# Running product on one Trainium2 core: where the square root's table is loaded, and where the second router's columns are copied

## What is computed

```python
mag = np.sqrt(a_re * a_re + a_im * a_im)
scale = np.minimum(mag, 0.999) / (mag + 1e-06)
a_re_n, a_im_n = (a_re * scale, a_im * scale)
for t in range(S):
    S_re, S_im = (ar * S_re - ai * S_im + kv, ar * S_im + ai * S_re)   # ar, ai: the decay of step t
    y[:, :, t] = np.einsum('bhd,bhde->bhe', q[:, :, t], S_re)
```

## Time and profile before

| | |
|---|---|
| three runs, median (lowest to highest) | 805.1 us (803.31 to 806.18) |
| profiled execution, its own time | 804.9 us |
| its span, first to last instruction | 803.0 us |
| mean granted TensorE clock | 0.951 |
| busy: PE, DVE, ACT, POOL | 700.5, 657.8, 476.1, 212.9 us |

### The profile page before, as it was taken

The page is one execution under the profiler, slowest core; times in us unless marked ns, Lnnn a source line. Parts: engine busy times, 40 slices in busy tenths (PEclk is TensorE's granted clock), DMA queues, the critical chain, the costliest instruction groups (busy, mean ns, idle before and its releaser), DMA issues.

```text
span 803.0 us, 17480 instructions
## 1 busy us (share of the span) xinstructions
PE 700.5 (87%) x6568; PEld 622.4 (78%) x6568; DVE 657.8 (82%) x1241; ACT 476.1 (59%) x660; POOL 212.9 (27%) x184
## 2 busy tenths in 40 slices
PE   0577867169999999947999999999999999999997
PEld 0323332158888888847999998998999999999997
DVE  7998999989999999967888767756898696676672
ACT  7678988566676676552656544646544545544541
POOL 3000000031111111105153566532344322233422
PEclk9888989579999999977999999999999999999999
DMA  7463643017853332455666866776565755756630
GB/s 192 152 216 124 207 161 109 0 34 147 158 145 101 108 118 89 166 116 177 203 220 202 278 222 205 238 222 219 192 216 180 265 192 191 245 208 188 245 139 30
DMA packets 90900, 136.85 MB, mean 170 GB/s; under 512 B 22474, under 2 KB 70070, under 8 KB 90656
## 3 DMA queue, kind: packets, MB, share of 16 engines
q1 hardware_dynamic: 83680, 119.54, 47.9%
q0 software_dynamic: 7168, 16.64, 5.8%
HBM read 124.15 MB, written 14.01 MB: 172 GB/s over the span
## 4 chain that ended last, share of the span: by engine, by line
PE 47%; DVE 4%; DMA 2%; issue 1%; ACT 1%; POOL 0%; POOLq 0%; SPq 0%; DVEq 0%
PE banks L1385 23%; PE banks L1342 22%; PE banks L1328 2%; DVE mix_spot L1578 1%; DVE w_lo L972 1%; DMA raw<-w1b 1%; DMA mix_rows<-xbuf,lists 1%; DVE mix_hT_lo L1677 0%; DMA xbuf<-mix_y,to_scatter 0%; PE banks L1320 0%; ACT mix_hT_hi L1425 0%; DVE mix_y L1701 0%; ACT w_hi L961 0%; POOL to_scatter L1218 0%; POOLq L1091 0%
## 5 line engine op out<-in xcount | busy, mean ns | idle before, releaser
L1342 PE MATMUL banks<-mix_xT_hi,w_hi 128*128 128x240 f32 x576 | 158.8, 276 | 0.6 <-DVE mix_xT_lo L1686 0.6
L1342 PE MATMUL banks<-mix_xT_lo,w_hi 128*128 128x240 f32 x576 | 158.9, 276 | 0.0
L1342 PE MATMUL banks<-mix_xT_hi,w_lo 128*128 128x240 f32 x576 | 158.8, 276 | 0.0
L1385 PE MATMUL banks<-w_hi,mix_hT_hi 128*128 128x384 f32 (+3 forms) x384 | 135.7, 353 | 3.8 <-DVE mix_hT_lo L1677 3.8
L1385 PE MATMUL banks<-w_lo,mix_hT_hi 128*128 128x384 f32 (+3 forms) x384 | 129.8, 338 | 0.0
L1385 PE MATMUL banks<-w_hi,mix_hT_lo 128*128 128x384 f32 (+3 forms) x384 | 129.7, 338 | 0.0
L1425 ACT ACTIVATE mix_hT_hi<-banks 128x480 fp32r<-128x480 f32 x96 | 54.8, 572 | 111.0 <-PE banks L1342 106.0
L1342 PEld LDWEIGHTS banks<-mix_xT_hi,w_hi 128*128 128x128 f32 x576 | 109.5, 190 | 0.9 <-issue 0.8
L1342 PEld LDWEIGHTS banks<-mix_xT_hi,w_lo 128*128 128x128 f32 x576 | 109.6, 190 | 0.0
L1342 PEld LDWEIGHTS banks<-mix_xT_lo,w_hi 128*128 128x128 f32 x576 | 109.5, 190 | 0.0
L1677 DVE SCALAR_TENSOR_TENSOR mix_hT_lo<-banks,mix_hT_hi 128x480 fp32r<-128x480 f32 x96 | 62.7, 653 | 50.5 <-ACT mix_hT_hi L1425 50.4
(11 more groups left out here) (230 smaller groups left out, 1469.0 us busy)
## 6 DMA issues: line engine op xcount, KB each, us to landing
raw<-w1b SPq DMA_DIRECT2D x16, 1536.0 KB, 7.9
raw<-w2b SPq DMA_DIRECT2D x16, 1536.0 KB
A<-w2a_t SPq DMA_DIRECT2D x8, 1536.0 KB, 8.4
raw<-w1a SPq DMA_DIRECT2D x8, 1536.0 KB
raw<-w2a SPq DMA_DIRECT2D x8, 1536.0 KB
ring<-a SPq DMA_DIRECT2D x9, 864.0 KB, 5.1
qk<-q SPq DMA_DIRECT2D x48, 96.0 KB, 2.3
qk<-k SPq DMA_DIRECT2D x48, 96.0 KB, 2.3
```

What stands on the lines that cost most here:

```text
L1342: last = pe.matmul(pU[g % TURNS][:, n * N:(n + 1) * N], w1p[m][:, b, c, f * P:(f + 1) * P], xT[s][:, c, 0:N], start=(c == 0 and (s, m) == ...
L1385: last = pe.matmul(pD[0:m, half, 0:ph.width], hT[s][:, f, half * P:half * P + m], w2p[w][:, b, f, 0:ph.width], start=(f == 0 and (s, w) == ...
```

## The change

The table set of the square root is asked for in the loop's text at each g from 0 to 9, behind `spread_out(g - 1)` and ahead of the waits in `roots(g + 2)`. The copy to `held` moves from g = 10, behind `negate(11)`, to g = 9, behind `negate(10)`. The copy to `scores` moves from g = 11, behind `spread_out(10)`, to g = 10, behind `spread_out(9)` and ahead of `negate(11)`. POOL's memset is cut into one of plane 1, which waits for the eight scores, and one of plane 0, which waits for the transposes as before.

```diff
-            sp.wait_ge(gap_set, 1)
+            sp.wait_ge(gap_set, 2)
...
+            pool.wait_ge(scored, E)
+            pool.memset(A[LANE1 // 2:LANE1, 1, PSEG:SEG, :], 1.0).then_inc(gap_set, 1)
             pool.wait_ge(scores_turned, 1)
-            pool.memset(A[LANE1 // 2:LANE1, :, PSEG:SEG, :], 1.0).then_inc(gap_set, 1)
+            pool.memset(A[LANE1 // 2:LANE1, 0, PSEG:SEG, :], 1.0).then_inc(gap_set, 1)
...
+            def hold_scores():
+                act.wait_ge(scored, E)
+                for n in range(E // QUADS):
+                    act.copy(held[:, n * F:(n + 1) * F].rearrange("p (h f) -> p h f", h=2),
+                             banks[:, 3 + 2 * n:5 + 2 * n, :]).then_inc(scores_held, 1)
+
+            def copy_scores():
+                act.wait_ge(scores_turned, 1)
+                for n in range(E // QUADS):
+                    last = act.copy(scores[:, n * QUADS:(n + 1) * QUADS].rearrange("p i c k -> p c i k"),
+                                    banks[:, 3 + 2 * n:5 + 2 * n, :].rearrange("p b (c i k) -> p (b c) i k", i=QUADS,
+                                                                               k=QUAD)[:, :, :, 0:E])
+                last.then_inc(scores_copied, 1)
...
                 if g > 0:
                     spread_out(g - 1)
+                if g + 2 < GROUPS:
+                    act.preload_act_table_set("sqrt_and_others")
                 if g == 0:
-                    act.preload_act_table_set("sqrt_and_others")
                     act.wait_ge(emb_step, 2)
                     act.activation(embn[:, 2:3], embn[:, 1:2], ACT.Sqrt).then_inc(emb_step, 1)
+                if g == GROUPS - 2:
+                    copy_scores()
                 if g + 2 < GROUPS:
                     roots(g + 2)
                     act.preload_act_table_set("natural_log_exp_and_others")
...
                 if EARLY + 2 <= g + 1 < GROUPS:
                     negate(g + 1)
-                if g == GROUPS - 2:
-                    act.wait_ge(scored, E)
-                    for n in range(E // QUADS):
-                        act.copy(held[:, n * F:(n + 1) * F].rearrange("p (h f) -> p h f", h=2),
-                                 banks[:, 3 + 2 * n:5 + 2 * n, :]).then_inc(scores_held, 1)
-                if g == GROUPS - 1:
-                    act.wait_ge(scores_turned, 1)
...
-                    last.then_inc(scores_copied, 1)
+                if g == GROUPS - 3:
+                    hold_scores()
             spread_last()
```

## The result

Five runs of the changed kernel gave 796.92 to 799.45 us, median 797.47; five of the kernel before, on the same chips, 801.23 to 806.18, median 803.31. The ratio is 0.9929 with a 95% interval of 0.9899 to 0.9958: faster by 0.7%, some 5.8 us by the medians. Forecast were 6.4 us and 798.7. The forecast time was worked out from 805.1, the median of the first three of those five runs before; with all five that median is 803.31. So the time came 1.2 us under the forecast although 0.6 us less was gained.

What follows compares the result with a forecast made beforehand. Stage 1's end was taken to count, with DVE's chain waiting for ACT and its last copy beside POOL's memset. 3.8 + 2.6 = 6.4 us off 804.9 gives 798.5, median 0.2 above: 798.7 us; range 797.4 to 802.4.

Steps and rivals of the forecast that it cites:

- Both parts, and that they add up: Stage 1: loads ahead of the waits give 3.8 us, the stage's end 2.6 us, together 6.4 us.
- The loads, 3.8 us: Stage 1, groups 4 and 5: square root table loads ahead of ACT's waits shorten DVE's waits, 3.8 us by group 5.
- Group 5: PE's sum takes 3.18 us, negate(5) ends at 72.43, DVE does not wait; gain by then 3.8 us, or 2.75.
- Rival 1: PE's sum of group 6 stays slow: 1.0 us less gain, 799.7 us; chance 0.68 together with the forecast.
- the fast sum: PE's sum after 1.3 us of idle time taken at 3.18 us, not 6.13 us.
- group 4: 1.28 us less between sum and negate(4), plus 0.15 us from an earlier load: 1.43 us; DVE's wait of 0.34 us stays.
- Groups 6 to 11, nothing: Stage 1 from group 6 on: moved loads gain nothing, as DVE bounds there and does not wait for negate(6).
- Copies to `held` and `scores` at no cost: ACT late in stage 1: its 2.03 us of idle time covers the 1.91 us copies to `held`; `scores` end long before negate(11).
- The end, 2.6 us: End of stage 1: without POOL's memset beside it DVE's last copy takes 0.32 us; DVE done 2.6 us sooner (2.2 to 2.75).
- The table's load: ACT: 1.28 us per load without the skill's 1380 ns drain; were the drain there and hidden, 0.3 us more gain.
- Rival 5: PE enters stage 2 cold after a 16 us gap; one unit costs up to 7.7 us, 808 us, say; chance 0.05.

Runs made afterwards that it cites:

- the two runs with one part each: Kernel before with the loads alone added: ratio 0.9957; changed kernel without the loads (early score copies, memset in two): ratio 0.9962.
- the first four runs: Loads alone on the kernel before, 0.9957; changed kernel without loads, 0.9962; with score copies where they were, 0.9939; with memset in one piece, 0.9923.

## Why the prediction was right, point by point

- *Both parts, and that they add up:* right, by the two runs with one part each.
- *The loads, 3.8 us:* 3.37 in the changed kernel, 3.65 with the loads alone. Group 5 came as worked out: fast sum, no wait. Rival 1 (the sum stays slow) did not show in any of the nine profiles with these loads where PE stood 1.5 us ahead of it; in the three without them it stood 2.77 us and the sum took 6.13, 4.77 and 4.59. The reason I gave, the shorter idle time, is not shown by that: in the same nine the next group's sum came behind 3.5 us of idle time and took 3.18 us in three and 4.59 to 6.13 in six, and in the profile before it took 3.18 behind 3.06. The choice of the fast sum was in part luck. The mis-sized term is group 4: 1.00 us for 1.43, because the first score, which I moved as it stood (7.42 us), took 8.00 at its clock. DVE kept a wait of 0.91 us, not 0.34. The forecast gain also rests on a wait at group 5 that was long in the profile before: 2.37 us, against 1.01 and 0.83 in the two other profiles without the loads. Over all profiles the gain holds even so: DVE's last copy starts at 161.03 to 162.39 us in the three profiles without the loads (mean 161.8) and at 157.40 to 159.02 in the eight with all of them and PE's old order (mean 158.3).
- *Groups 6 to 11, nothing:* right with all loads. That their loads themselves are worth nothing is not quite so: 0.34 us at group 6 when a sum is slow.
- *Copies to `held` and `scores` at no cost:* right, 0.22 us of wait left in front of `spread_out(9)`, as against some 0.1 forecast.
- *The end, 2.6 us:* from the copy's start to the end of the small writes it was 3.32 us and is 0.83, so 2.49. The copy takes 0.42 alone, not 0.32. The cause, POOL's memset, stands by three runs: two inputs free it, a later memset holds it again, an earlier one of either shape lets it go. The rule in the Trainium skill (SBUF — State Buffer, Who interferes with whom) told each of these rightly, the two-input case beside a memset (0.69 us) among them. Of the second part's two edits the cut of the memset is enough alone (its end and the copy's start then lie 0.12 us apart), and so is moving the copies.
- *The table's load:* every load had 1.28 us, and the one at 66.52 starts as the copy ends and the root follows at 67.82. The second term that the Trainium skill gives (ScalarE: Activation LUTs, What ACT_TABLE_LOAD costs), 1380 ns of drain, shows in none of these profiles.
- *Rival 5, a cold start of stage 2:* did not happen, though by little: in the first profile of the changed kernel the 28 transposes took 6.17 us and PE stood 0.53 us ahead of its first work, with the clock at 0.95 in that microsecond. That need not be the moved copies' doing, as the run with two loads, with the score transposes where they were, had the same 0.53 us. The price I gave, up to 7.7 us for a unit, was 6.0 where the run with 14 transposes paid it; the 9 us in that rival's sum had no row behind it.

## What to carry to other kernels

A load or a short job that needs nothing from the wait belongs ahead of it, but its worth is only what the bounding engine still waits for there: nine loads moved, and two of them paid 3.3 of 3.65 us. At a stage's end look at every engine's last item, side work too: here a filler memset on GpSimd, needed by nobody until stage 2, held a 0.4 us copy on VectorE for 2.5 us; cutting it in two or running it earlier freed the copy, while writing the copy with two inputs only passed the hold on to the next writes. And where a stage's length varies from run to run by a microsecond, read it from the trace, at the start of the next stage.

## What the runs showed of the hardware that was not expected

- The hold reaches small operations: four one-input writes of 60 elements stood for the memset as the copy had, 2.27 us in place of 0.48. A copy that begins 0.12 us ahead of the memset's end took no longer than one alone (0.41 us).
- The same 28 transposes took between 4.56 and 6.18 us, and not by how long PE had stood: 4.56, 4.95 and 6.18 us behind 6.46 us of idle time, 5.54 behind 3.96, 5.61 behind 6.00, 5.01 to 6.17 behind some 15.8, 5.08 behind 17.44. What I had expected of the idle time in the first four runs was wrong; when the clock rises within a burst stays open.
- A two-input operation that copies transposed took 0.69 us for 288 elements beside the memset, where a plain one in the first microseconds of the kernel takes 0.46. Whether the order of the elements or the memset makes the difference was not tried.
